# Transposes on TensorE replaced by 32x32 block turns on VectorE, with h sent through DRAM, in a three-stage attention and expert kernel

## The chip, the cores and the metric

One core of one Trainium2 chip. The metric is the device time of one execution in microseconds, the median of several runs. A profiled execution of the same program gives the trace that is read here.

## The reference, cut to what matters

Block-sparse attention (2 batches, 8 heads, 768 positions, heads of 64) gives 1536 tokens of 512 numbers. A gate picks one of eight experts for each token, and the token goes through that expert's two layers. Last comes a dense layer pair with a squared ReLU.

```
logits = x @ w_gate + modality_bias[modality_id]
e_idx  = argmax(logits);  gate_w = softmax(logits)[e_idx]
for e in range(8):
    h = maximum(x[mask] @ w1[e], 0)          # 512 -> 1024
    out[mask] = gate_w[mask] * (h @ w2[e])   # 1024 -> 512
h = maximum(x @ w_in, 0)                     # 512 -> 2048
return h * h @ w_out                         # 2048 -> 512
```

## The kernel before, in words

**Attention** runs over 12 blocks of 128 tokens. Its rows are scattered to DRAM (xs_d), sorted by expert. With these inputs three experts have tokens, in 13 tiles of 128 rows.

**Expert tiles.** Every product is made of three fp32r matmuls: each operand is split into a high part, rounded by a copy on ScalarE (x_hi, h_hi, W), and a low part, the rest, from a subtraction on VectorE (x_lo, h_lo). Layer 1 is 24 matmuls of 512 columns into banks 0 and 1 (lines 1536 to 1538), layer 2 is 24 matmuls into bank 4 (lines 1559 to 1561). Tiles 0 to 2 are written out ahead of the loop, tiles 3 to 12 run in a loop over pairs. TensorE's order in the loop is: layer 1 of tile t; 4 transposes of x for tile t+1 (`x_transpose`, line 1492, from x_in to bank 5); layer 2 of tile t-1; 8 transposes of h for tile t (`h_transpose`, line 1569, banks 2 and 3).

ScalarE's order in a step is: ReLU of the two halves of h (line 673), x_hi of t+1, h_hi twice (line 677), the store of y of tile t-1 (line 688), and last, at some tiles, the splitting of the next weights, whose turn it reads from a table in SBUF (`split_next`; one half of 2 MB at a time, four copies of 1024 columns). VectorE's order: x_lo of t+1, copy of y(t-1) out of bank 4 (line 1179), h_lo twice, low parts of the weights (`low_next`). GpSimd loads the weights, 2 MB at a time, and makes two of a run's eight low parts. SyncE loads x tile by tile (`load_x`). All engines take their instructions in this order and wait on semaphores: `x_t` counts turned x tiles, `ht` turned halves of h, `hh` and `hl` their high and low parts, `relu` the ReLUs, `y` the copies of y, `l1` and `l2` the finished layers.

**Dense layers.** Rows come back from DRAM (ys_d) in three groups of 512. The first group's rows (z) are scaled by the gate weight and turned by 16 TensorE transposes between the last h_transpose and the last expert layer 2 (`part_transposes`). Inside a group, `up(g, f)` is 12 matmuls for 128 of the 2048 hidden columns and `down(g, f)` 12 matmuls back, two steps behind. The next group's z is scaled on VectorE in the middle of a group and turned by 8 transposes after the last `up` and 8 after the next `down` (`z_transpose`, line 1633). 24 more matmuls of `down` end the group, and the four results are copied to o_sb and scattered to the output.

Of the kernel before, what the change touches and what calls it, by code (L numbers as in the profile page):

```python
# [14 lines left out]
P = 128  # L15
# [36 lines left out]
GT = 4  # L52
# [16 lines left out]
AHEAD = 1  # L69
VPITCH = 9 * P  # L70
# [74 lines left out]
def build(nc, a):  # L145
# [26 lines left out]
    cursor["t"] = c_mark + (2 * DM + 2 * DM + FE + 2 * FE + 2 * DM + DM) * 4  # L172
# [96 lines left out]
    x_hi = sb("c", "x_hi", [P, KD, P], F32R)  # L269
    x_lo = sb("c", "x_lo", [P, KD, P], F32R)  # L270
    h_sb = sb("c", "h_sb", [P, FE], F32)
    h_hi = sb("c", "h_hi", [P, KF, P], F32R)
    h_lo = sb("c", "h_lo", [P, KF, P], F32R)
# [8 lines left out]
    z_in = sb("c", "z_in", [P, GT, DM], F32)  # L282
# [9 lines left out]
    z_part = [sb("c", f"z_part{s}", [P, DM], F32) for s in range(2)] + x_in  # L292
    z_hi = sb("c", "z_hi", [P, KD, GT * P], F32R)
    z_lo = sb("c", "z_lo", [P, KD, GT * P], F32R)

# [5 lines left out]
    ys_d = nc.dram_tensor("ys_d", (N + P, DM), F32).ap()  # L301
    meta_d = nc.dram_tensor("meta_d", (N, 2), F32).ap()
# [17 lines left out]
    def Wv(slot, lo, col, n):  # L320
# [10 lines left out]
        raw0 raw1 zfill scat_a x_t x_h x_l l1 relu ht hh hl l2 y sh sla slbv slbp  # L331
        counts both ylast wo_h wo_v zin scale zt zh zl m1 r sqs s_h s_l mo o_a o_v out ofree den_ok""".split()
# [10 lines left out]
    s_part = [nc.alloc_semaphore(f"s_part{j}") for j in range(GT)]  # L343
# [60 lines left out]
    def part_bank(j):  # L404

        return bank[(6, 7, 0, 1)[j]]

    def z_bank(k):

        return bank[6 + k % 2]  # L410

    block = nc.Block()
    with block:

        @block.sync
        def _(sp):
# [69 lines left out]
            def load_x(t, s):  # L486
                row = sp.value_load(table[0:1, bass.ds(t + T_ROW, 1)], min_val=0, max_val=E * EROWS)
                sp.dma_start(x_in[s][:, :], xs_d[bass.ds(row, P), :]).then_inc(s_xs[s], 16)
# [24 lines left out]
            sp.wait_ge(sem["tab"], 1)  # L513
            done = sp.value_load(table[0:1, T_DONE:T_DONE + 1], min_val=LEAST - RECENT, max_val=TILES - RECENT)
            for s in range(2):
                stored = sp.snap(((done + (RECENT - s)) >> 1) * 16)
                sp.wait_ge(s_ys[s], stored)
            sp.wait_ge(sem["metas"], NB * 16)
            for j in range(GT):
                if j == 2:  # L520
                    sp.wait_ge(sem["x_t"], n_t + 1)
                sp.dma_start(z_part[j][:, :], ys_d[j * P:(j + 1) * P, :]).then_inc(s_part[j], 16)
# [7 lines left out]
            sp.sem_inc(sem["ofree"], 1)  # L530
            for g in range(1, GROUPS):
                sp.wait_ge(sem["zt"], g * KD)
                sp.dma_start(z_in[:, :, :], ys_d[g * GT * P:(g + 1) * GT * P, :].rearrange("(j p) d -> p j d", p=P)
                             ).then_inc(sem["zin"], 16)
# [7 lines left out]
        def _(act):  # L542
# [45 lines left out]
            def x_high(t):  # L588
                act.wait_ge(sem["x_t"], t + 1)
                act.activation(x_hi[:, :, :], x_bank(t)[:, :].rearrange("p (k t) -> p k t", k=KD), ACT.Copy  # L590
                               ).then_inc(sem["x_h"], 1)
# [37 lines left out]
            def split_next(t, half):  # L629

                k = act.value_load(table[0:1, bass.ds(t + T_NEXT, 1)], min_val=0, max_val=E)
                with act.If(k > 0):
                    split_w(act.value_load(table[0:1, bass.ds(t + T_NEXT, 1)], min_val=1, max_val=E), half)
# [26 lines left out]
            def parts_high():  # L660
                for j in range(GT):
                    act.wait_ge(sem["zt"], j + 1)
                    act.activation(z_hi[:, :, j * P:(j + 1) * P], part_bank(j)[:, :].rearrange("p (k t) -> p k t", k=KD),
# [1060 lines left out]
```

## Time and the profile before

| what | us |
|---|---|
| median of 3 runs | 521.39 (521.07 to 522.05) |
| profiled execution, its own time | 521.77 |
| span of its instructions | 520.1 |
| TensorE busy | 508.1 (98%) |
| VectorE busy | 225.4 (43%) |
| ScalarE busy | 188.0 (36%) |
| GpSimd busy | 87.1 (17%) |
| mean granted TensorE clock | 0.998 |

Busy shares are averages over the whole span, and the attention, expert and dense stages have different work. The chain that ended last is 95% TensorE.

### The profile page before, as it was taken

To read this page: it belongs to the slowest core of one execution; us is meant where nothing else is said; L and a number is where in the kernel's file an instruction comes from. 1 tells how busy PE (TensorE), PEld (TensorE's weight loads), DVE (VectorE), ACT (ScalarE), POOL (GpSimd) and SP (SyncE) were. 2 spreads that over 40 slices of the span, in tenths; PEclk is the share of its full clock that TensorE was granted. 3 is DMA by queue.
4 is the path that set the end of the run, shared out by engine and by line. 5 is a ranking of instruction groups with operands and counts; after the bars stand their busy time and mean duration, and the time that the engine had idled before them with its cause. 6 is when DMAs were issued, how large, how long until landed. Compare 5 with 4: busy or idle time off the path is not lost.

```text
span 520.1 us, 9415 instructions
## 1 busy us (share of the span) xinstructions
PE 508.1 (98%) x3115; PEld 410.0 (79%) x3117; DVE 225.4 (43%) x440; ACT 188.0 (36%) x355; POOL 87.1 (17%) x110
## 2 busy tenths in 40 slices
PE   8889999999999999999999999999999999999995
PEld 3678788888888888888788888888888888888884
DVE  4787686974323554237632422342242233222221
ACT  1876665243524544225522212331221233122121
POOL 4434335027600223100000000300000020000002
PEclk9999999999999999999999999999999999999999
DMA  8999666384661655521200000400000020000002
GB/s 285 336 290 340 235 220 228 99 285 104 189 216 41 219 204 202 202 82 40 83 1 1 0 1 0 161 0 0 0 0 0 0 81 0 0 0 0 0 0 81
DMA packets 19018, 54.92 MB, mean 106 GB/s; under 512 B 2848, under 2 KB 3120, under 8 KB 18480
## 3 DMA queue, kind: packets, MB, share of 16 engines
q1 hardware_dynamic: 11200, 27.47, 16.6%
q0 software_dynamic: 5200, 23.62, 12.6%
q10 hardware_dynamic: 2592, 3.49, 1.8%
q8 instruction: 15, 0.25, 0.2%
q14 instruction: 11, 0.09, 0.1%
HBM read 42.51 MB, written 12.07 MB: 105 GB/s over the span
## 4 chain that ended last, share of the span: by engine, by line
PE 95%; DVE 3%; issue 1%; ACT 1%; POOL 0%; POOLq 0%; DVEq 0%; ACTq 0%
PE psum L1653 9%; PE psum L1654 9%; PE psum L1652 9%; PE psum L1668 8%; PE psum L1669 8%; PE psum L1670 8%; PE psum L1536 5%; PE psum L1559 5%; PE psum L1538 5%; PE psum L1560 5%; PE psum L1561 5%; PE psum L1537 5%; PE psum L1396 2%; PE psum L1569 2%; PE psum L1371 2%; PE psum L1456 2%
## 5 line engine op out<-in xcount | busy, mean ns | idle before, releaser
L1326 DVE TENSOR_TENSOR sq<-r_sb 128x512 f32<-128x512 f32 x48 | 33.2, 692 | 141.4 <-ACT r_sb L734 137.4
L734 ACT ACTIVATE r_sb<-psum 128x512 f32<-128x512 f32 x48 | 28.7, 597 | 143.7 <-PE psum L1654 143.7
L1668 PE MATMUL psum<-W,s_hi 128*128 128x512 f32 x192 | 75.9, 395 | 0.1
L1653 PE MATMUL psum<-z_lo,W 128*128 128x512 f32 x192 | 75.8, 395 | 0.0
L1654 PE MATMUL psum<-z_hi,W 128*128 128x512 f32 x192 | 75.8, 395 | 0.0
L1652 PE MATMUL psum<-z_hi,W 128*128 128x512 f32 x192 | 75.8, 395 | 0.0
L1669 PE MATMUL psum<-W,s_hi 128*128 128x512 f32 x192 | 75.5, 393 | 0.0
L1670 PE MATMUL psum<-W,s_lo 128*128 128x512 f32 x192 | 75.4, 393 | 0.0
L893 POOL DMA_INDIRECT out<-o_sb,sorted_m x12 | 11.6, 969 | 293.5 <-DVE o_sb L1342 291.6
L1328 DVE TENSOR_TENSOR s_lo<-sq,s_hi 128x512 fp32r<-128x512 f32 x48 | 33.2, 692 | 33.5 <-ACT s_hi L736 33.5
L736 ACT ACTIVATE s_hi<-sq 128x512 fp32r<-128x512 f32 x48 | 30.3, 632 | 41.8 <-DVE sq L1326 41.8
L1668 PEld LDWEIGHTS psum<-W,s_hi 128*128 128x128 f32 x192 | 36.1, 188 | 8.7 <-issue 0.5
L1652 PEld LDWEIGHTS psum<-z_hi,W 128*128 128x128 f32 x192 | 36.0, 188 | 8.7
L1654 PEld LDWEIGHTS psum<-z_hi,W 128*128 128x128 f32 x192 | 36.0, 187 | 8.7
L1653 PEld LDWEIGHTS psum<-z_lo,W 128*128 128x128 f32 x192 | 36.0, 188 | 8.6
L1670 PEld LDWEIGHTS psum<-W,s_lo 128*128 128x128 f32 x192 | 36.1, 188 | 8.2
L1669 PEld LDWEIGHTS psum<-W,s_hi 128*128 128x128 f32 x192 | 36.1, 188 | 8.1
L1536 PE MATMUL psum<-W,x_hi 128*128 (+1 forms) x104 | 42.1, 405 | 0.3 <-DVE x_lo L1018 0.3
L1559 PE MATMUL psum<-W,h_hi 128*128 (+1 forms) x104 | 42.0, 404 | 0.0
L1538 PE MATMUL psum<-W,x_lo 128*128 (+1 forms) x104 | 40.9, 393 | 0.0
L1560 PE MATMUL psum<-W,h_hi 128*128 (+1 forms) x104 | 40.9, 393 | 0.0
L1561 PE MATMUL psum<-W,h_lo 128*128 (+1 forms) x104 | 40.7, 391 | 0.0
(205 smaller groups left out, 729.5 us busy)
## 6 DMA issues: line engine op xcount, KB each, us to landing
raw<-in_w POOLq DMA_DIRECT2D x4, 2048.0 KB, 9.1
raw<-in_w_io POOLq DMA_DIRECT2D x4, 2048.0 KB, 8.2
v_in<-in_v SPq DMA_DIRECT2D x12, 390.0 KB, 12.7
raw<-in_w SPq DMA_DIRECT2D x8, 512.0 KB, 4.3
kT<-in_kT SPq DMA_DIRECT2D x8, 400.0 KB, 7.9
q_in<-in_q SPq DMA_DIRECT2D x12, 256.0 KB, 8.8
X<-in_vT SPq DMA_DIRECT2D x4, 768.0 KB, 11.7
x_in<-xs_d SPq DMA_DIRECT2D x12, 256.0 KB, 2.8
```

Of the source, the lines that this page charges most:

```text
L1326: dve.tensor_tensor(sq[:, :], r_sb[:, :], r_sb[:, :], ALU.mult).then_inc(sem["sqs"], 1)
L1536: pe.matmul(bank[h][:, :], x_hi[:, k, :], wh, start=(k == 0), stop=False)
L1538: ins = pe.matmul(bank[h][:, :], x_lo[:, k, :], wh, start=False, stop=(k == KD - 1))
L1559: pe.matmul(bank[4][:, :], h_of(t)[1][:, k, :], wh, start=(k == 0), stop=False)
L1560: pe.matmul(bank[4][:, :], h_of(t)[1][:, k, :], wl, start=False, stop=False)
L1561: ins = pe.matmul(bank[4][:, :], h_lo[:, k, :], wh, start=False, stop=(k == KF - 1))
L1652: pe.matmul(bank[f % 2][:, :], wh, z_hi[:, k, :], start=(k == 0), stop=False)
L1653: pe.matmul(bank[f % 2][:, :], wh, z_lo[:, k, :], start=False, stop=False)
L1654: ins = pe.matmul(bank[f % 2][:, :], wl, z_hi[:, k, :], start=False, stop=(k == KD - 1))
L1668: pe.matmul(bank[2 + j][:, :], s_hi[f % SBUFS][:, tok], wh, start=(f == 0), stop=False)
L1669: pe.matmul(bank[2 + j][:, :], s_hi[f % SBUFS][:, tok], wl, start=False, stop=False)
L1670: ins = pe.matmul(bank[2 + j][:, :], s_lo[f % SBUFS][:, tok], wh, start=False, stop=(f == KFF - 1))
```

## The change

- **x in the loop** (tiles 4 to 13): the load from xs_d puts quarter q of the columns on partitions 32q to 32q+31, four tokens to a partition (pieces of 512 B). One VectorE instruction turns all 16 blocks of 32x32 into x_w, which lies where x_lo will be. x_hi and x_lo are made from x_w. There is no TensorE transpose.
- **h in the loop** (tiles 3 to 11): after each ReLU half, SyncE writes the half to DRAM (h_d) and reads it back in the other layout (`spread_h`); VectorE turns it into h_w, which lies where h_lo will be; then h_hi and h_lo. The first half may be turned when half of layer 2 of t-1 is through (`l2m`), the second when all of it is. The last tile and tiles 0 to 2 keep TensorE's transposes.
- **Order**: on ScalarE the splitting of weights stands between x_hi and h_hi, and the second-half split waits for layer 2 of t-1. On VectorE the weights' low parts stand before the turn of h, and the copy of y(t-1) after h_lo. Layer 2 alternates between banks 4 and 7 and takes h by halves.
- **z**: loaded in the same layout in four DMAs per group, turned by four VectorE instructions per group after the last `up`, with z_hi and z_lo from the turned copy in SBUF. The gate weight is no longer applied to z; its square (g_sq) scales the last copies to o_sb.
- **Weights**: the rows of w1, w2 and w_in are laid out in another order ahead of the launch, since a turned tile has column 4p+k of its input on partition p. The TensorE transposes that stay read every fourth column accordingly.

```diff
@@ sync
+            def spread_h(t, lap):
+                for h in range(2):
+                    sp.wait_ge(sem["relu"], t * 2 + (h + 1))
+                    sp.dma_start(h_d[h].rearrange("q t f -> t q f"),
+                                 h_sb[:, h * DM:(h + 1) * DM].rearrange("t (q f) -> t q f", q=KD)).then_inc(s_hd[h], 16)
+                for h in range(2):
+                    sp.wait_ge(s_hd[h], lap * 16)
+                    sp.dma_start(h_q[h][:, :], h_d[h].rearrange("q (a j) f -> (q a) (j f)", a=QW)).then_inc(s_hq[h], 16)
...
                     moe_step(t + 1, 0)
+                    spread_h(t, m * 2 + 1)
+                    with sp.If(t + 2 == n_t):
+                        load_parts()
+            def load_z(g, into):
+                for q in range(KD):
+                    sp.dma_start(into[q * QW:(q + 1) * QW, :], quarter(ys_d[g * GT * P:(g + 1) * GT * P, :], q)
+                                 ).then_inc(sem["zin"], 16)
@@ scalar, split_next
+                    k = act.value_load(table[0:1, bass.ds(t + T_NEXT, 1)], min_val=1, max_val=E)
+                    if seconds is not None:
+                        act.wait_ge(sem["l2"], seconds)
+                    split_w(k, half)
@@ scalar, moe_step
                 x_high(t + 1)
+                if not isinstance(t, int):
+                    with act.If(t == last):
+                        parts_high()
+                    split_next(t - 1, 1, t)
+                    split_next(t, 0)
...
+                    with act.If(t < last):
+                        for h in range(2):
+                            act.wait_ge(sem["ht"], t * 2 + (h + 1))
+                            act.activation(h_hi[:, 4 * h:4 * h + 4, :], h_w[:, 4 * h:4 * h + 4, :], ACT.Copy
+                                           ).then_inc(sem["hh"], 1)
...
-                if not isinstance(t, int):
-                    split_next(t - 1, 1)
-                    split_next(t, 0)
@@ vector
+            def x_turn(t, s, lapx):
+                dve.wait_ge(s_xs[s], lapx * 16)
+                dve.wait_ge(sem["l1"], t * 2)
+                dve.transpose(turned(x_w[:, :, :]), blocks(x_in[s][:, :])).then_inc(sem["x_t"], 1)
+
+            def h_turn(t, h, lap):
+                dve.wait_ge(s_hq[h], lap * 16)
+                dve.wait_ge(sem["l2" if h else "l2m"], t)
+                dve.transpose(turned(h_w[:, 4 * h:4 * h + 4, :]), blocks(h_q[h][:, :])).then_inc(sem["ht"], 1)
...
+            def loop_step(t, s, lap):
+                with dve.If(t == last):
+                    parts_turn()
+                x_turn(t + 1, s, lap + 1)
+                x_low(t + 1, True)
+                low_next(t - 1, range(PARTS, PARTS + 2))
+                low_next(t, range(PARTS))
+                with dve.If(t == last):
+                    z_low(0)
+                    h_low(t)
+                with dve.If(t < last):
+                    for h in range(2):
+                        h_turn(t, h, lap * 2 - 1 + s)
+                        h_low(t, (h,), True)
+                dve.wait_ge(s_ys[s], lap * 16 + 16)
+                y_copy(t - 1, y_sb[s], s)
+                with dve.If(t == last):
+                    out_low(range(PARTS))
+                    y_copy(last, y_last, 1 - s)
...
                 with dve.If(g < GROUPS - 1):
-                    z_low(g + 1)
+                    dve.wait_ge(sem["zin"], (g + 2) * (KD * 16))
+                    dve.wait_ge(sem["m1"], g * KFF + KFF)
+                    z_turn(z_in, 0)
+                    for k in range(KD):
+                        if k + 1 < KD:
+                            z_turn(z_in, k + 1)
+                        z_low(g + 1, (k,))
                     dve.wait_ge(sem["mo"], g * GT + (j + 1))
-                    dve.tensor_copy(o_sb[:, j, :], bank[2 + j][:, :]).then_inc(sem["o_v"], 1)
+                    dve.tensor_scalar(o_sb[:, j, :], bank[2 + j][:, :], g_sq[:, bass.ds(g * GT + j, 1)], None, ALU.mult
+                                      ).then_inc(sem["o_v"], 1)
@@ tensor, layer2
+                if not isinstance(t, int) or t > 1 - AHEAD:
+                    pe.wait_ge(sem["y"], t - 1 + AHEAD)
...
+                    if k == KF // 2 - 1:
+                        ins.then_inc(sem["l2m"], 1)
@@ tensor, loop
-            def moe_step(t, s, lapx):
+            def moe_step(t, s):
                 last = []
                 layer1(t, *weights_of(t), between=((KD // 2, lambda: last.extend(weights_of(t - 1))),))
-                x_transpose(t + 1, s, lapx)
-                layer2(t - 1, *last)
-                h_transpose(t)
+                layer2(t - 1, s, *last)
...
-                    if f == KFF - 1:
-                        with pe.If(g < GROUPS - 1):
-                            z_transpose(g + 1, range(2))
```

## Rows read from the trace of the kernel before

**Rows 1.** The page: busy us, share, instructions; busy tenths; granted TensorE clock in tenths.

```profile
PE 508.1 (98%) x3115; PEld 410.0 (79%) x3117; DVE 225.4 (43%) x440; ACT 188.0 (36%) x355; POOL 87.1 (17%) x110
...
PE   8889999999999999999999999999999999999995
...
PEclk9999999999999999999999999999999999999999
```

**Rows 2.** Groups of TensorE: line, op, shapes, count, busy us, mean ns.

```profile
L1569 PE MATMUL psum<-ident,h_sb 128*128 128x128 f32 x104 | 13.5, 272 | 0.0
```

**Rows 3.** Chain that ended last, expert loop: start, us, what.

```profile
116.84 0.44 PE psum L1492 x4
...
154.14 0.44 PE psum L1492 x4
...
160.10 0.87 PE psum L1569 x8
...
172.44 0.87 PE psum L1569 x8
```

**Rows 4.** The same chain at the first border of two groups.

```profile
323.88 0.87 PE psum L1633 x8
327.51 1.03 PE psum L1633 x8
```

**Rows 5.** Timeline at that border.

```profile
325.94 0.69 DVE L1328 TENSOR_TENSOR s_lo<-sq,s_hi 128x512 fp32r<-128x512 f32 x1 [0.70 <-ACT s_hi L736]
```

**Rows 6.** The chain before the last expert layer 2.

```profile
234.13 0.88 PE psum L1569 x8
...
237.14 0.36 PE psum L1559
```

**Rows 7.** Timeline at the same place.

```profile
235.24 1.29 DVE L1013 TENSOR_TENSOR h_lo<-psum,h_hi 128x512 fp32r<-128x512 f32 x2 [0.30 <-ACT h_hi L677]
...
236.36 1.09 ACT L663 ACTIVATE z_hi<-psum 128x512 fp32r<-128x512 f32 x2 [0.66 <-PE psum L1621]
```

**Rows 8.** Timeline of ScalarE, tiles 5 to 7.

```profile
154.67 0.59 ACT L590 ACTIVATE x_hi<-psum 128x512 fp32r<-128x512 f32 x1
160.57 1.09 ACT L677 ACTIVATE h_hi<-psum 128x512 fp32r<-128x512 f32 x2 [5.31 <-PE psum L1569]
161.85 0.35 ACTq L688 DMA_DIRECT2D ys_d<-y_sb  x1
164.54 3.90 ACT L585 ACTIVATE W<-raw 128x1024 f32 x4 [2.88 <-issue]
...
176.37 3.90 ACT L585 ACTIVATE W<-raw 128x1024 f32 x4 [2.37 <-issue]
```

**Rows 9.** Timeline of VectorE, tiles 6 and 7.

```profile
160.20 0.69 DVE L1179 COPY y_sb<-psum 128x512 f32<-128x512 f32 x1 [4.21 <-PE psum L1561]
161.20 1.29 DVE L1013 TENSOR_TENSOR h_lo<-psum,h_hi 128x512 fp32r<-128x512 f32 x2 [0.31 <-ACT h_hi L677]
165.88 4.63 DVE L1005 TENSOR_TENSOR W<-raw,W 128x1024 f32 x4 [3.39 <-ACT W L585]
...
177.77 2.36 DVE L1005 TENSOR_TENSOR W<-raw,W 128x1024 f32 x2 [2.94 <-ACT W L585]
```

**Rows 10.** DMA issues, KB each, us to landing; last line: loads of x_in.

```profile
raw<-in_w POOLq DMA_DIRECT2D x4, 2048.0 KB, 9.1
...
ys_d<-y_last SPq DMA_DIRECT2D x1, 256.0 KB, 2.1
...
DMA to landing us min/median/max: 2.5/2.8/4.1
```

**Rows 11.** Groups of VectorE, columns as in rows 2.

```profile
L1309 DVE TENSOR_SCALAR z_in<-z_in,sorted_m 128x512 f32<-128x512 f32 x8 | 3.3, 481 | 0.0
```

**Rows 12.** Timeline of GpSimd: weight loads in the loop, first and last of six.

```profile
134.99 0.81 POOL L849 DMA_DIRECT2D raw<-in_w  x1 [0.46 <-issue]
...
210.22 0.57 POOL L858 DMA_DIRECT2D raw<-in_w_io  x1 [0.41 <-issue]
```

More of the change, by code:

```diff
@@ L342, in build @@
     s_ys = [nc.alloc_semaphore(f"s_ys{s}") for s in range(2)]
[L343 removed]
+    s_hd = [nc.alloc_semaphore(f"s_hd{h}") for h in range(2)]
+    s_hq = [nc.alloc_semaphore(f"s_hq{h}") for h in range(2)]
     s_wo = [nc.alloc_semaphore(f"s_wor{s}") for s in range(2)]
@@ L487, in load_x, with load_parts @@
                 row = sp.value_load(table[0:1, bass.ds(t + T_ROW, 1)], min_val=0, max_val=E * EROWS)
-                sp.dma_start(x_in[s][:, :], xs_d[bass.ds(row, P), :]).then_inc(s_xs[s], 16)
+                if isinstance(t, int) and t <= SPEC:
+                    sp.dma_start(x_in[s][:, :], xs_d[bass.ds(row, P), :]).then_inc(s_xs[s], 16)
+                else:
+                    sp.dma_start(x_in[s][:, :], xs_d[bass.ds(row, P), :].rearrange("(a j) (q f) -> q a j f", a=QW, f=P)
+                                 ).then_inc(s_xs[s], 16)
+            def spread_h(t, lap):
[10 more added lines that the diff above has]
+                                 ).then_inc(sem["zin"], 16)
+            def load_parts():
+                sp.wait_ge(sem["tab"], 1)
+                done = sp.value_load(table[0:1, T_DONE:T_DONE + 1], min_val=LEAST - RECENT, max_val=TILES - RECENT)
+                for s in range(2):
+                    stored = sp.snap(((done + (RECENT - s)) >> 1) * 16)
+                    sp.wait_ge(s_ys[s], stored)
+                sp.wait_ge(sem["metas"], NB * 16)
+                load_z(0, z_q)
             sp.wait_ge(sem["scat_b"], RGROUPS[2][1] * 16)
@@ L510, in _ @@
                     moe_step(t + 1, 0)
+                    spread_h(t, m * 2 + 1)
+                    with sp.If(t + 2 == n_t):
+                        load_parts()
                     with sp.If(t + 2 < n_t):
                         moe_step(t + 2, 1)
[L513 to L522, printed above, removed]
+                        spread_h(t + 1, m * 2 + 2)
+                        with sp.If(t + 3 == n_t):
+                            load_parts()
             at = sp.value_load(table[0:1, bass.ds(n_t - 1 + T_POS, 1)], min_val=0, max_val=N)
@@ L660, in parts_high @@
             def parts_high():
-                for j in range(GT):
-                    act.wait_ge(sem["zt"], j + 1)
-                    act.activation(z_hi[:, :, j * P:(j + 1) * P], part_bank(j)[:, :].rearrange("p (k t) -> p k t", k=KD),
-                                   ACT.Copy).then_inc(sem["zh"], 1)
+                act.wait_ge(sem["zt"], KD)
+                for k in range(KD):
+                    act.activation(z_hi[:, k, :], z_w[:, k, :], ACT.Copy).then_inc(sem["zh"], 1)
             def moe_step(t, s=None, before=None):
@@ L1552, in layer2 @@
                             do()
-                    if halves and k == KF // 2:
+                    if k == KF // 2:
                         pe.wait_ge(sem["hl"], t * 2 + 2)
```

207 lines of the change are left out of this document (99 added, 108 removed).

## The prediction

> **What bounds the kernel now.** Page first, then the chain, then TensorE's, ScalarE's and VectorE's timelines in the expert loop, then the transfers. The page [rows 1] has TensorE busy for 508.1 us of the span at full granted clock (tenths of 9 throughout: the 2.4 GHz level), VectorE for 225.4, ScalarE for 188.0. The chain stays on TensorE through the loop: between two groups of transposes lie 24 matmuls, 154.58 to 160.10, so a layer is 5.52 us (0.23 per matmul), and a tile is 4 transposes of x (0.44), layer 2 of the tile before, 8 transposes of h (0.87), layer 1: 12.34 us [rows 2, 3]. (Matmul rows of 0.39 overlap; the distance of starts is the price.) Nothing on the other engines is late there: ScalarE and VectorE wait for TensorE (5.31 us before h_hi, 4.21 before the copy of y) [rows 8, 9]. So each TensorE instruction removed is worth its time, as long as what replaces it keeps under TensorE's other work.
>
> **What is removed.** Tiles 3 to 12 run in the loop (13 tiles: 104 transposes of h are 13 times 8 [rows 2]). Ten turns of x go, 10 x 0.44 = 4.4 us; nine of h (tiles 3 to 11; the last tile keeps TensorE's), 9 x 0.87 = 7.8. The 32 transposes of z at the two group borders are 0.87 + 1.03 each border, 2 x 1.90 = 3.8 us [rows 4]; the 16 before the last layer 2 occupy the 2.13 us between the end of h's transposes (235.01) and that layer's start (237.14) [rows 6]. If all that replaces them were hidden: at the last place h_lo's first half ends only at 235.93, so 0.9 of the 2.13 stays as a wait [rows 7], and 4.4 + 7.8 + 1.2 + 3.8 = 17.2 us are saved.
>
> **Group borders.** After the last first-layer matmul of a group TensorE still has 36 matmuls (8.3 us). VectorE must do sq and s_lo (2.8 us after it: 326.63, where the transposes behind those matmuls are through from 323.88 on [rows 4, 5]), then 4 turns and 4 subtractions at some 0.65 us: 8.1 us for all four quarters, while next group's matmuls want them at 8.3, 9.0, 9.7, 10.4. Even turns of 1.2 us fit nearly (10.4). The z rows are asked for a whole group ahead. I count the full 3.8. The factor g squared in the last copies replaces copies of the same shape: nothing.
>
> **The new ring.** The loop is another matter. ScalarE and VectorE work in order, and in ScalarE's order the ReLU of tile t+1 stands behind the store of y(t-1), which waits for VectorE's copy of y(t-1), which now stands behind both halves of h(t): turn, h_hi, h_lo. Those wait for h(t)'s trip through DRAM, which starts at the ReLU of tile t. So from ReLU to ReLU there is a ring that TensorE's 11.0 us per tile (24 + 24 matmuls) doesn't enter. Its prices: x_hi 0.6, and the ReLU, a copy of the same shape, the same [rows 8]; h_hi 0.58 with 0.08 to hand over; h_lo and y copies 0.64 apiece in a row (1.29 for two) [rows 9]. The transfers: 256 KB took 2.1 us out (y_last), 2.5 to 4.1 in, median 2.8 [rows 10]. The write out has pieces of 512 B, which no row shows; bounds 2.1 and 4.1, I take 2.7 for it, near the store with its larger pieces, and 2.7 for the way back. The 32x32 turn isn't shown either: 0.48 (the scale of z_in, SBUF to SBUF) below, 1.2 (the 128x1024 subtraction, 2.36 for two) above [rows 9, 11]; I take 0.64, the in-a-row price of the other 128x512 instructions.
>
> Plain tile, counted from the start of its ReLU: ReLU 0.6, issue 0.15, out 2.7, 0.05, back 2.7, 0.1: h's first half is back at 6.3. Turn 0.64, h_hi 0.66, h_lo 0.72: 8.3. The second half, already there, the same in order: 10.3. Copy of y 11.0; store's issue and the loop's edge (0.1 + 0.35 + 0.5): the next ReLU at **11.9**. TensorE needs 11.0. So each plain tile gets 0.9 later than TensorE's pace, which by itself would take 2.9 us of slack first.
>
> **Tiles that split weights.** Before, the splits stood behind h_hi and the store; now they stand ahead of h_hi on ScalarE and ahead of the turn on VectorE. First half of a run's weights (tiles 6, 8): ReLU pair and x_hi are done at 1.7, the table reads take 2.34 (162.20 to 164.54), and VectorE's fourth part ends 5.97 after the first of ScalarE's starts (164.54 to 170.51) [rows 8, 9]: 10.0. The trip is covered, but then turn, h_hi, h_lo (2.0) twice, copy and edge follow: **15.7**. Second half (tiles 7, 9): reads 1.76, VectorE's two parts end 3.76 after the start: 7.2, ring **12.8**. Tile 3 splits a second half too and ScalarE waits there for layer 2's end at 5.5, then 3.9 of copies: ring 14.9.
>
> Six weight loads of 2 MB (9.1 us each) fall between 134.99 and 218 [rows 10, 12]. An x load issued in such a load took up to 4.1 instead of 2.7. I add 0.6 per transfer, 1.2 per trip, where the trip is what the ring waits for: tiles 4, 5, 11. Bounds 0 and 2.8.
>
> **The sum**, from the end of layer 1 of tile 3. ReLU(3) -0.5; +14.9 tile 3; +13.1 +13.1 tiles 4, 5; +15.7 +12.8 +15.7 +12.8 tiles 6 to 9; +11.9 tile 10: ReLU(11) at 109.5. Tile 11's copy of y ends 11.0 + 1.2 later, 121.7. In the last tile VectorE turns z's four quarters first (2.6), then x of the unused tile 13 (0.74), then ScalarE x_hi (0.7), four z_hi (2.07, as 1.09 for two in [rows 7]), two table reads (1.76), h_hi 0.6, h_lo 0.7: the last layer 2 starts at 130.9. Before, it was 237.14 - 116.84 = 120.3 [rows 3, 6] on the same scale (19 layers of 5.52, 10 x 0.44, 10 x 0.87, 2.13). So +10.6, less 3.8 at the borders: **+6.8 us**. Against the profiled execution's 521.77 (0.4 above the median of 521.39) that is 528.6; I forecast **528.5**.
>
> With every price at its lower bound (2.1 and 2.5 for the trip, no contention, turns 0.48): rings of tiles 4, 5, 10, 11 lose 0.8 each, contention 3.6, 23 turns 0.16 each: 10.5 less, 518. If table reads and the loop's edge run ahead behind ScalarE's work as well (some 0.6 x 5 + 0.3 x 9), 512. Upper: both transfers 4.1 adds 2.8 to four rings, less the 3.6 counted: +8; turns of 1.2 add 23 x 0.56 = 13: 550.
>
> The turns read and write fp32 values 16 bytes apart. Only contiguous 128x512 rows stand in this trace, at 0.48 to 0.69 us [rows 9, 11]. The Trainium skill ("SBUF — State Buffer", Door 1: The DMA port swizzle) says that SBUF serves lines of 16 bytes and that a stream that moves to a new line at each access pays for it; no run here shows it yet. By it the turn lies at the upper bound, and the 48 TensorE transposes that stay, which now read with that step too, would also cost more. That outcome is the second rival.
>
> **The rivals.**
> - *The ring is short* (chance 0.17, other side): trips of 4.6 us and run-ahead reads give 512 to 518; if no ring binds at all, 521.8 - 17.2 = 504.6. For it: the quickest landings are 2.1 and 2.5, and VectorE is idle for over half of a plain tile. Against: splits now stand ahead of h even then, and two rings of over 15 us stay. It decides where the summed rings fall 6.8 us below mine, a plain ring of 11.0 or less with splits of 14.5.
> - *Turns are slow* (0.15): 1.2 us each, 528.6 + 13 = 542; 48 transposes at twice their 0.11 would add 5.
> - *The trip is slow* (0.10): landings near 4 us, 536 to 538.
> - *The gaps let TensorE's clock fall* (0.03): gaps of 1 to 5 us per tile would come; the trace of before has no slice in which TensorE is busy under 0.8 up to the last, so it shows no clock after such gaps [rows 1]. A fall to the 1.2 GHz level would double the following 5.52 us layers: above 550.
> - *Tie by accident* (0.05).
> The forecast itself (528.5, own range 522.5 to 535): 0.50.
>
> **How the numbers follow.** Within 0.2% (1.04 us) is what a measurement of this kernel can't tell from no change. Faster 0.18, same 0.05, slower 0.77. Range 514 to 544: it takes in the short ring at its bounds and the slow turns, and leaves out the fully hidden case and the clock.
>
> **What would show it.** Gaps of TensorE before layer 2 of tiles 4 to 11, ended by h_lo; ReLUs that start 11 to 16 us apart, ended by the store of y or a wait on VectorE; landings of about 2.7 for h_q; a TRANSPOSE row of about 0.65 on VectorE; ScalarE's h_hi idle until a turn. At the borders, up-matmuls with no wait and a group 1.9 us shorter. Wrong if ReLU to ReLU is 11.0 in plain tiles (TensorE still sets the pace), or if the turn is over 1 us.

## The result and the profile after

The changed kernel takes 565.98 us (median of 4 runs, 564.26 to 569.31) against 521.72 for the kernel before on the same chip (521.07 to 523.8): ratio 1.085, 95% interval 1.0817 to 1.0884. Forecast were 528.5, slower, with 514 to 544 as the range. So the direction came as forecast, and the loss is 44 us where 6.8 were counted. Some executions of a kernel take over 1.5% longer than its fastest; the ratios below leave these out, the medians don't.

The page of the changed kernel, cut to what answers to [rows 1]: busy us and share; busy tenths of TensorE; granted clock in tenths; the chain by engine.

```profile
PE 505.8 (90%) x2956; PEld 403.4 (72%) x2957; DVE 267.1 (47%) x469; ACT 190.7 (34%) x355; POOL 88.7 (16%) x110
...
PE   7999999994579775788499999999999999999995
...
PEclk9999999996979797889889999999999999999998
...
PE 61%; DMA 18%; DVE 7%; issue 4%; ACT 4%; ACTq 2%; SPq 1%; DVEq 1%; POOL 0%; POOLq 0%
```

TensorE has 159 instructions fewer than before and is busy only 2.3 us less, because matmuls at a low clock last longer. The damage is in slices 10 to 20 (127 to 282 us), the expert loop: busy tenths of 4 to 8 in all but one of them where [rows 1] has 9, and the granted clock falls in most of them. TensorE's waits in the loop (110 to 290 us; who waited for whom, us in total, times, longest) name one thing:

```profile
PE psum L1640 <- DVE h_lo L1076: 42.1, 8, 9.2
PE psum L1616 <- DVE x_lo L1083: 4.0, 5, 1.1
```

L1640 is the first matmul of layer 2. The chain shows what stands behind h_lo. Tiles 3 and 4 first, then tile 5, in which no weight load runs:

```profile
117.47 0.49 ACT h_sb L718
...
118.52 8.49 DMA h_d<-h_sb
127.03 8.05 DMA h_q<-h_d
135.10 1.14 DVE h_w L1093
136.26 0.64 ACT h_hi L740
...
137.55 0.69 DVE y_sb L1253
138.48 0.34 ACTq L751
...
139.52 0.60 ACT h_sb L718
140.14 8.82 DMA h_d<-h_sb
148.98 6.14 DMA h_q<-h_d
...
162.08 0.61 ACT h_sb L718
162.70 2.35 DMA h_d<-h_sb
165.08 2.60 DMA h_q<-h_d
```

This is the ring of the prediction, link by link: ReLU, out, back, turn, h_hi, h_lo, copy of y, its store, next ReLU. The quiet trip is 2.35 + 2.60 (counted: 2.7 + 2.7). The other two are 16.5 and 15.0. ReLU to ReLU takes 22.1, 22.6, 12.2, 16.2, 15.6, 18.3, 17.6, 16.1 and 12.3 us in tiles 3 to 11: 153.1 together, 123.1 forecast.

The turns of h among VectorE's groups in the loop (columns as in [rows 2]); the ten of x have a mean of 1118 ns:

```profile
L1093 DVE STREAM_TRANSPOSE h_w<-h_q 128x512 f32<-128x512 f32 x18 | 20.1, 1117 | 34.7 <-DMA h_q<-h_d 34.6
```

Stretches of the trace (start and end, us, busy time and count of each engine, granted clock, DMA share, GB/s): the write of tile 3, the layer 2 behind its trip, the writes of tiles 4 and 5, the last layer 2, and the second MLP:

```profile
118.50:127.00 8.50, 7.91 (x35) 6.21 (x34) 4.86 (x5) 4.54 (x5) 6.67 (x7) 1.00 0.51 105
135.40:140.40 5.00, 5.00 (x12) 3.94 (x13) 3.21 (x4) 1.51 (x3) 4.11 (x4) 0.50 0.41 62
140.10:149.00 8.90, 8.39 (x35) 6.52 (x35) 2.53 (x1) 1.02 (x3) 4.39 (x4) 0.96 1.01 366
162.70:165.10 2.40, 2.40 (x12) 1.97 (x11) 0.69 (x1) 0.98 (x2) 0.00 (x0) 1.00 0.57 174
283.00:287.00 4.00, 4.00 (x10) 3.14 (x11) 1.43 (x3) 2.34 (x3) 0.00 (x0) 0.50 0.17 66
300.00:540.00 240.00, 240.00 (x1037) 194.32 (x1036) 80.27 (x111) 63.73 (x104) 7.78 (x8) 1.00 0.05 14
```

Tile 4's long write has the DMA engines full, with two weight loads of 2 MB issued at 137.54 and 144.61. In its first 5.4 us (140.1 to 145.5) the queues moved (packets, MB, share of the engines' time; q0 has GpSimd's loads, q1 SyncE's pieces of h):

```profile
q0 software_dynamic: 399, 1.63, 81.3%
...
q1 hardware_dynamic: 60, 0.03, 1.9%
```

From 145.5 to 149 q1 moves 0.49 MB. So the write hardly moves before 1.6 MB of the loads have moved. Tile 8's is the same (0.01 MB in the first 5.0 us), and tile 10's too (none in the first 3.4). Tile 3's is another case: q1 moves 0.48 MB in 4.0 us and needs another 4.5 for 0.12 MB, at 29 GB/s in all, while GpSimd's scatters are on their way.

And the last tile, where z is turned ahead of h (the chain of the changed kernel; it answers to [rows 6]):

```profile
265.75 5.91 DMA z_q<-ys_d
271.68 0.06 DVE z_w L1320
...
272.73 3.05 DVE z_w L1320 x3
...
281.81 0.61 DVE h_lo L1076
...
282.86 0.79 PE psum L1640
```

The last layer 2 starts at 282.86, 45.7 us later than in [rows 6]. From there to the end of the span the changed kernel needs 281.2, the one before 283.0. So all of the loss lies ahead of this point.

### The profile page after: what moved, and what is told of

The parts are those of the page before. It is cut to its first block, busy times and chain, and to the rows that moved or that the text cites. A ratio compares the mean times of both kernels' runs of the same rounds, so it can differ in the third digit from the quotient of the medians.

```text
span 564.1 us, 9300 instructions
## 1 busy us (share of the span) xinstructions
PE 505.8 (90%) x2956; PEld 403.4 (72%) x2957; DVE 267.1 (47%) x469; ACT 190.7 (34%) x355; POOL 88.7 (16%) x110
## 4 chain that ended last, share of the span: by engine, by line
PE 61%; DMA 18%; DVE 7%; issue 4%; ACT 4%; ACTq 2%; SPq 1%; DVEq 1%; POOL 0%; POOLq 0%
PE psum L1717 8%; PE psum L1718 8%; PE psum L1716 8%; PE psum L1733 8%; PE psum L1732 8%; PE psum L1734 8%; DMA h_d<-h_sb 7%; DMA h_q<-h_d 4%; DVE h_w L1093 3%; DMA q_in<-in_q 3%; PE psum L1640 2%; ACT h_hi L740 2%; PE psum L1641 1%; PE psum L1642 1%; PE psum L1450 1%
## 5 line engine op out<-in xcount | busy, mean ns | idle before, releaser
L1640 PE MATMUL psum<-W,h_hi 128*128 (+1 forms) x104 | 48.4, 465 | 42.1 <-DVE h_lo L1076 42.1
L794 ACT ACTIVATE r_sb<-psum 128x512 f32<-128x512 f32 x48 | 28.7, 597 | 145.8 <-PE psum L1718 139.6
L954 POOL DMA_INDIRECT out<-o_sb,sorted_m x12 | 11.6, 966 | 309.5 <-DVE o_sb L1420 307.0
L1640 PEld LDWEIGHTS psum<-W,h_hi 128*128 128x128 f32 x104 | 23.0, 221 | 51.1 <-issue 45.9
L1641 PE MATMUL psum<-W,h_hi 128*128 (+1 forms) x104 | 46.0, 442 | 0.0
L1642 PE MATMUL psum<-W,h_lo 128*128 (+1 forms) x104 | 45.6, 438 | 0.0
## 6 DMA issues: line engine op xcount, KB each, us to landing
v_in<-in_v SPq DMA_DIRECT2D x12, 390.0 KB, 12.2
```

Source lines behind the costliest of these rows:

```text
L1640: pe.matmul(y, h_of(t)[1][:, k, :], wh, start=(k == 0), stop=False)
L1641: pe.matmul(y, h_of(t)[1][:, k, :], wl, start=False, stop=False)
L1642: ins = pe.matmul(y, h_lo[:, k, :], wh, start=False, stop=(k == KF - 1))
```

## The experiments

Each kernel is the changed one with the edit shown, unless said otherwise. The ratio is to the kernel before, run in turn with it on the same chip. Where effects are compared in us, the ratio is taken times 521.7; the changed kernel is then 566.0.

**The trip and the traffic beside it**

*Loads cut.*

```diff
-                    pool.dma_start(raw[:, part]...(k f)..., w[bass.ds(e, 1)]...)
+                    pool.dma_start(raw[:, part]...(k f)...[:, 0:1, :], w[bass.ds(e, 1), :, 0:1, :]...)
```

> Leaves out seven eighths (layer-2 halves) or three quarters (layer-1 halves) of each weight load inside the loop, so later experts and the dense pair compute with stale weights; nothing else differs from the changed kernel. Theory A (the loop's time is the sum of rings from ReLU to ReLU, and a ring is long where h's trip through DRAM runs beside another transfer): the trips of tiles 4, 8, 9, 10 fall from 8 to 15 us to about 5 us, and the time from 566 to about 548. The trip of tile 3 stays near 16 us, since the weight load beside it ended at 122.2 and the metadata scatters run to 135. Rival B (the weight loads don't matter, TensorE's fallen clock or VectorE's turns cost the time): 562 to 566.

549.06 us, ratio 1.0519 (1.0468 to 1.0571): 17 us less than the changed kernel. Tile 3's trip in its chain:

```profile
122.05 5.54 DMA h_d<-h_sb
127.61 5.05 DMA h_q<-h_d
```

10.6 instead of 16.5, where it was expected to stay near 16, and still twice the quiet one, though only a quarter or an eighth of a half's weights moves.

*No scatters.* The metadata scatters of GpSimd, which in the changed kernel run from 112.7 to 129.7, are replaced by one plain copy.

> Leaves out the 12 scatters of gate weight and token number to DRAM and their read back; the unsorted values are copied instead, so rows leave with another token's place and weight. Theory A (any transfer beside it lengthens the trip): the trip of tile 3, 16.5 us beside these scatters of 8-byte pieces, falls by some 8 us, and the time to about 558. Rival E (tile 3's trip is long because the weight load of 109.1 is still on its way): 564 to 566.

559.17 us, 1.0719 (1.068 to 1.0757), 7 us less. Tile 3's trip is 4.71 + 7.60: 4.2 less, where some 8 were expected. The run isn't clean. The loads that GpSimd issues behind the scatters, at 137.54 and 144.61 in the changed kernel, are issued at 123.96 and 135.16 here, so one of them falls on tile 3's way back, and the largest gain is in tile 4, where no scatters ran (from ReLU to ReLU 16.8 for 22.6). Both the loads and the scatters lengthen the trip of tile 3, by 6 and 4 us in one trace each; how the 7 us divide between the scatters themselves and the earlier loads isn't shown.

*x loads in four parts.*

```diff
-                    sp.dma_start(x_in[s][:, :], xs_d[bass.ds(row, P), :].rearrange("(a j) (q f) -> q a j f", a=QW, f=P)
-                                 ).then_inc(s_xs[s], 16)
+                    for q in range(KD):
+                        sp.dma_start(x_in[s][q * QW:(q + 1) * QW, :], quarter(xs_d[bass.ds(row, P), :], q)
+                                     ).then_inc(s_xs[s], 16)
```

> The x loads of the loop, in the changed kernel one transfer with 4 as its outermost dimension, are issued as four, one per quarter; the bytes are the same. In the changed kernel the DMA share stands at 0.25 for 8.3 us behind such a load (4 engines of 16) and at 0.55 to 0.72 in h's own transfers. Theory F (these 8 us on four engines lie before h's write in part of the tiles and hold it up beside a weight load): the long trips of tiles 4, 9 and 10 shrink by 2 to 4 us each, 555 to 560. Rival (weight loads alone make the trips long): 564 to 567.

567.47 us, 1.0845 (1.0814 to 1.0876): no change, so nothing shows that the x loads delay the trip. The time from ReLU to ReLU is spread otherwise, though: 28.7 us in tile 3 (22.1 in the changed kernel) and 19.3 in tile 4 (22.6). VectorE's and GpSimd's timelines in tile 3 show a second thing that the prediction hadn't; behind them stand two rows of the kernel before:

```profile
139.50 5.29 DVE L1077 TENSOR_TENSOR h_lo<-h_w,h_hi 128x512 fp32r<-128x512 f32 x1 [0.70 <-ACT h_hi L741]
139.53 4.70 POOL L891 TENSOR_TENSOR W<-raw,W 128x1024 f32 x2
```

```profile
179.67 5.09 POOL L829 TENSOR_TENSOR W<-raw,W 128x1024 f32 x2 [7.56 <-ACT W L585]
181.76 0.69 DVE L1018 TENSOR_TENSOR x_lo<-psum,x_hi 128x512 fp32r<-128x512 f32 x1 [1.63 <-ACT x_hi L590]
```

A subtraction of VectorE with both inputs in SBUF that starts beside one of GpSimd's ends some 0.55 us after it or its successor has ended (here 144.79, GpSimd's pair 144.23), and takes 0.8 to 5.3 us instead of 0.69. One with an input in PSUM takes 0.69 there, too. The change moved h and x from PSUM to SBUF. In the trace of the changed kernel three of the 18 h_lo and one of the ten x_lo are lengthened so, by 4.4 us together and up to 1.8 each, in the steps of tiles 4, 7 and 9; in the kernel before none is.

*Larger pieces out.*

```diff
-                    sp.dma_start(h_d[h].rearrange("q t f -> t q f"), h_sb[...].rearrange("t (q f) -> t q f", q=KD))
+                    sp.dma_start(h_d[h], h_sb[:, h * DM:(h + 1) * DM])
...
-                    sp.dma_start(h_q[h][:, :], h_d[h].rearrange("q (a j) f -> (q a) (j f)", a=QW))
+                    sp.dma_start(h_q[h][:, :], h_d[h].rearrange("(a j) (q f) -> q a j f", a=QW, f=P))
```

> h is written to DRAM in pieces of 2 KB (one row of a half) and read back in pieces of 512 B, the other way round than in the changed kernel; the result is the same. Theory A1 (a transfer in small pieces gets few turns beside another queue's large pieces, whichever way it goes): the long landings move from the write to the read, time 560 to 568. Rival A2 (it is writing 512 B pieces to DRAM that is slow): the trips beside weight loads shrink by some 4 us each, 548 to 555.

598.84 us, 1.1471 (1.1424 to 1.1517): 32 us worse, against both theories. Its chain in a tile without a weight load, and the stretch of the read-back by itself (columns as in the stretches above):

```profile
178.16 2.21 DMA h_d<-h_sb
180.39 8.37 DMA h_q<-h_d
```

```profile
180.40:189.00 8.60, 5.85 (x26) 4.51 (x25) 2.04 (x3) 0.63 (x1) 0.00 (x0) 1.00 0.25 71
```

With nothing beside it the write in whole rows is about as fast as the one in 512 B pieces (2.35), so there the size of the pieces isn't the price. The read now has an outermost dimension of 4 and uses a quarter of the DMA engines (share 0.25, 71 GB/s) for 8.4 us. The Trainium skill (DMA: Bandwidth & Descriptors, Rules for kernel authors) says that an outermost dimension smaller than 16 confines a transfer to at most that many engines; the 0.25 agrees. The run says little of contention, since it brought in a cost of its own; its writes in whole rows still took 4.3 to 9.9 us in tiles 4 and 7 to 10.

*No trip.* h is turned from where ReLU leaves it; its values then stand in other places.

```diff
-                dve.wait_ge(s_hq[h], lap * 16)
+                dve.wait_ge(sem["relu"], t * 2 + (h + 1))
                 dve.wait_ge(sem["l2" if h else "l2m"], t)
-                dve.transpose(turned(h_w[:, 4 * h:4 * h + 4, :]), blocks(h_q[h][:, :])).then_inc(sem["ht"], 1)
+                dve.transpose(turned(h_w[:, 4 * h:4 * h + 4, :]), blocks(h_sb[:, h * DM:(h + 1) * DM])).then_inc(sem["ht"], 1)
```

> Leaves out h's way through DRAM: VectorE turns h's blocks straight from h_sb (the blocks are then in the wrong partitions, so h is wrong), all waits and the order of the engines stay. Theory A: plain rings fall under TensorE's 11.0 us, only the rings with a first-half weight split (16 us) and the last tile still cost; about 521 us. Rival C (VectorE with turns of 1.12 us is the bound whatever the transfers do): 540 or more.

532.3 us, 1.0203 (1.0173 to 1.0233). The trip is worth 34 of the 44 us. But 521 was expected, and 10.6 us of loss remain without it. TensorE's waits in its loop:

```profile
PE psum L1634 <- DVE h_lo L1070: 14.4, 5, 5.0
```

Its rings are 10.6 to 10.8 in three tiles and 12.1 in tile 4, but 14.5 to 15.7 in the five tiles that split weights. That ring doesn't contain the trip.

*Splits behind h.* The same, with `split_next` and `low_next` put behind h_hi and h_lo.

```diff
                 x_low(t + 1, True)
-                low_next(t - 1, range(PARTS, PARTS + 2))
-                low_next(t, range(PARTS))
...
                         h_low(t, (h,), True)
+                low_next(t - 1, range(PARTS, PARTS + 2))
+                low_next(t, range(PARTS))
                 dve.wait_ge(s_ys[s], lap * 16 + 16)
```

> The changed kernel without the trip through DRAM (h turned from where ReLU writes it, so its values stand in other places), and with the splits of the next weights put behind the turns and splits of h on ScalarE and VectorE rather than ahead of them. It tells what the 10.5 us are that the kernel without the trip still lost. Theory (the order of the queues: a first-half split stands ahead of h_hi and h_lo and makes the ring 15.7 rather than 10.6 to 12): four such tiles by some 3.4, so 13 to 14 less than without the trip alone, 518 to 521, with the last ReLU of the loop near 227. Rival (TensorE needs the split halves as early as the turned h, so the wait moves from h_lo to the split weights): within 3 of the kernel without the trip, 529 to 533, with waits of layer 1 on the weights' low parts in the rows.

529.55 us, 1.012 (1.0074 to 1.0165): by the ratio 4 us less, where the theory said 13 and the rival under 3 (529 to 533). TensorE's waits:

```profile
PE psum L1610 <- DVE x_lo L1077: 8.7, 2, 4.7
PE psum L1634 <- DVE h_lo L1070: 3.4, 1, 3.4
```

The wait for h_lo is gone from the loop (the 3.4 left are at the last tile). Of the 9.3 us that it had there, 6.6 came back one step later, in front of layer 1, for x_lo (8.7 for 2.1). VectorE's timeline in such a tile says why:

```profile
185.53 1.12 DVE L1082 STREAM_TRANSPOSE x_w<-x_in 128x512 f32<-128x512 f32 x1
188.29 1.92 DVE L1077 TENSOR_TENSOR x_lo<-x_w,x_hi 128x512 fp32r<-128x512 f32 x1 [1.64 <-ACT x_hi L628]
190.13 1.09 DVE L1087 STREAM_TRANSPOSE h_w<-h_sb 128x512 f32<-128x512 f32 x1
...
197.20 4.64 DVE L1060 TENSOR_TENSOR W<-raw,W 128x1024 f32 x4 [2.17 <-ACT W L619]
201.75 0.68 DVE L1247 COPY y_sb<-psum 128x512 f32<-128x512 f32 x1
202.35 1.11 DVE L1082 STREAM_TRANSPOSE x_w<-x_in 128x512 f32<-128x512 f32 x1
```

A tile with a first-half split has x's turn and split, h's two turns and splits, four low parts and a copy of y on VectorE, with hand-overs to ScalarE between. From turn of x to turn of x that row of work takes 16.8 us (1.2 of them because x_lo runs beside GpSimd), and TensorE needs 11. In either order the tiles with a first-half split take 15.7 to 17.2. The rival had its number, but the waits are for x_lo and not for the weights' low parts, so neither theory had this: the order chiefly chooses where it is felt.

**VectorE's part of the ring**

*Copy of y ahead.*

```diff
+                dve.wait_ge(s_ys[s], lap * 16 + 16)
+                y_copy(t - 1, y_sb[s], s)
                 with dve.If(t < last):
                     for h in range(2):
                         h_turn(t, h, lap * 2 - 1 + s)
                         h_low(t, (h,), True)
-                dve.wait_ge(s_ys[s], lap * 16 + 16)
-                y_copy(t - 1, y_sb[s], s)
```

> The copy of y of tile t-1 stands ahead of the turn of h instead of behind h_lo; the result is the same. Theory A: ScalarE's store no longer waits for the second h_lo and the copy, 1.4 to 1.8 us less per ring, nine rings: about 552. Rival D (the ring closes only through the transfers and the buffer of h, not through ScalarE's store): 566 unchanged.

561.07 us, 1.075 (1.0722 to 1.0778): 5 us, where 14 were expected. It takes the tail off the ring in plain tiles (11.0 and 10.7 for 12.2 and 12.3), but the waits for h_lo stay at 41.4 us, and tiles 3 and 4 still take over 21 us. The nine rings are 7.5 shorter in its trace, and the last tile, up to layer 2, 1.4 longer (13.8). The h_hi of a tile stands ahead of the next ReLU on ScalarE in any case, and that waits for the trip. In two places its chain goes over TensorE instead: h_lo, layer 2, and then what waits for that layer (once the turn of the next tile's h, once a second-half split). So cutting the ring at the copy of y leaves others of nearly the same length.

*Contiguous turns.* x and h are turned block by block in place, so their values stand in other places; z's turns stay.

```diff
-                dve.transpose(turned(h_w[:, 4 * h:4 * h + 4, :]), blocks(h_q[h][:, :])).then_inc(sem["ht"], 1)
+                dve.transpose(h_w[:, 4 * h:4 * h + 4, :].rearrange("p k (n c) -> p (k n) c", c=QW),
+                              h_q[h][:, :].rearrange("p (n c) -> p n c", c=QW)).then_inc(sem["ht"], 1)
```

> The turns of x and h on VectorE read and write contiguous values instead of one value every 16 bytes (the elements then land in other places, so the result is wrong); instruction count, sizes and waits are the changed kernel's, z's turns stay as they are. If the 16-byte step costs: a turn falls from 1.12 to some 0.65 us, two turns per ring and one more in the last tile, about 9 us less: 556. If the block turn itself costs 1.12 us for 512 columns: 566.

561.24 us, 1.0782 (1.0712 to 1.0851): 3.5 us less, with an interval of 0 to 7, where 9 were expected. The turn by itself is clear:

```profile
L1094 DVE STREAM_TRANSPOSE h_w<-h_q 128x512 f32<-128x512 f32 x18 | 12.7, 707 | 36.5 <-DMA h_q<-h_d 36.5
...
L1322 DVE STREAM_TRANSPOSE z_w<-z_q 128x512 f32<-128x512 f32 x4 | 4.1, 1101 | 2.9 <-DMA z_q<-ys_d 2.9
```

Contiguous 0.71, with the 16-byte step 1.12: the step costs 0.41. The 0.64 of the prediction was near the contiguous one. The rule that the prediction cited from the Trainium skill (SBUF — State Buffer, Door 1) agrees in direction.

**The clock**

*Fillers.* Twenty bf16 matmuls of 512 columns that nobody uses, before each layer 2 of the loop.

```diff
+                for _ in range(20):
+                    pe.matmul(bank[6]..., fill[:, 0:P], wide(fill[:, :], 1, 2), start=True, stop=True)
                 layer2(t - 1, s, *last)
```

> 20 bf16 matmuls of 512 columns (0.23 us each, 4.6 us) on a spare bank stand between layer 1 and layer 2 of every tile of the loop; the result is the same. They keep TensorE at work for half of the long gaps. Theory A (TensorE isn't in the ring, so a slow layer 2 mostly costs slack): granted clock above 0.98 in the loop, but the time moves by less than 5 us, 561 to 570. Rival B (the 16 us by which the layer 2 matmuls are longer add to the time): 550 to 553.

569.87 us, 1.0904 (1.0833 to 1.0975), by the ratio 3 more than the changed kernel; the mean granted clock is 0.99 instead of 0.955. The first of the three matmuls of its layer 2, with TensorE's wait:

```profile
L1642 PE MATMUL psum<-W,h_hi 128*128 (+1 forms) x85 | 37.4, 440 | 12.3 <-DVE h_lo L1078 12.3
```

TensorE waits 30 us less (the fillers stand in the gaps), its matmuls are half to two thirds of the way back to the price of the kernel before (475, 452 and 447 ns became 440, 412 and 413; before 403, 394 and 391), and the time doesn't fall. The rival's 550 to 553 is out: most of what layer 2 loses to the clock is slack. It isn't quite nothing. The second-half split waits for layer 2, and in tile 7 of the changed kernel the chain runs through that layer (186.42 to 194.77), with its first matmuls 0.43 apart; the split's low parts end 1.1 us later than forecast. There the fillers take as much time as they can give back, so this run doesn't measure it.

**The versions with h on TensorE**

*Hybrid.* h goes back to TensorE's transposes and the order of the kernel before; x and z stay on VectorE.

> h goes back to TensorE's transposes and the weight splits back behind the store, x and z stay turned on VectorE. Theory A: no ring is left, 4.4 us of x transposes and 3.8 us of z transposes are saved and some of the 2.1 us before the last layer 2: 512 to 514. Rival C (a turn of 1.12 us per tile on VectorE delays the splits or x_lo): 519 to 523.

522.79 us, 0.999 (0.9958 to 1.0023): even, the number of the rival. Its chain at the last tile (z's load lands at 227.4):

```profile
229.35 2.05 DVE z_w L1306 x2
231.41 0.98 DVE x_w L1078
...
237.82 0.49 PE psum L1626
```

The last layer 2 starts at 237.82, later than the 237.14 of [rows 6]: z's turns stand before x and h on VectorE. The loop ahead of it gained nothing either: the last ReLU is at 227.68 against 227.53. A plain tile takes 11.96 instead of 12.34, so a turn of x does save some 0.4, but the first tiles of the loop give it back, where TensorE waits 0.9 for x_lo and 1.6 for nothing that the profile shows.

*Order of the last tile.* The hybrid, with z turned and split after h.

```diff
                 with dve.If(t == last):
-                    parts_turn()
...
                 h_low(t)
                 with dve.If(t == last):
+                    parts_turn()
+                    z_low(0)
                     out_low(range(PARTS))
```

> As h1_hybrid, but in the last tile h_hi and h_lo stand ahead of the turn and the split of z's first group. In h1_hybrid the last layer 2 started at 237.8 (before: 237.1), after a wait of 3.0 us on h_lo behind z's turns, whose rows landed only at 227.4, and TensorE's clock fell after it. Theory G (x and z on VectorE save what was counted, 4.4 and 3.8 us, and h1_hybrid gave it back at this one place): 515 to 518. Rival C (the turns of x cost elsewhere): 521 to 523.

527.05 us, 1.0081 (1.0034 to 1.0129): slower than the hybrid, where 515 to 518 were expected. Layer 2 does start sooner, 8.4 us after the last ReLU instead of 10.1. Then TensorE waits 0.8 for z_lo and 4.2 for the first ReLU of the dense layers, which ScalarE starts late:

```profile
254.93 0.60 ACT L781 ACTIVATE r_sb<-psum 128x512 f32<-128x512 f32 x1 [5.82 <-DVE g_sq L1372]
```

g_sq is the gate's square, one instruction of 0.17 us. ScalarE waits for it ahead of all dense layers, and VectorE makes it only behind z, the weights' low parts and the last copy of y. After this gap the granted clock is 0.50 (255.6 to 260.0). The same wait of 5.8 stands in the next two versions. So the theory isn't refuted: these runs measure the place of g_sq along with the order, and one with g_sq made earlier wasn't run.

*The same with x on TensorE.*

> As h3_order, but x too is turned by TensorE as in the kernel before; only z's turns are on VectorE. Theory G: 4.4 us more than h3_order, 519 to 522. Rival (x's turns on VectorE give nothing, since splits and x_lo wait behind them): equal to h3_order within 1 us.

528.45 us, 1.0119 (1.0067 to 1.0172). Against 527.05 of the run before, x on VectorE is worth 1.4 us, within the spread of both.

*The same with x loads in four parts.*

> h3_order with the x loads by quarters. With no trip in the ring, x loads are covered by a whole tile: equal to h3_order within 1 us (both theories); over 2 us less would say that the 8 us loads also hold up the store of y and z's rows at the end.

525.56 us, 1.0049 (1.0013 to 1.0086): the interval overlaps that of the version without it. Not settled.

*Borders alone.* The kernel before, with nothing of the loop touched:

```diff
-                with dve.If(g < GROUPS - 1):
-                    z_low(g + 1)
+                with dve.If(g < GROUPS - 1):
+                    dve.wait_ge(sem["zin"], (g + 1) * (KD * 16))
+                    dve.wait_ge(sem["m1"], g * KFF + KFF)
+                    z_turn(z_in, 0)
+                    ...
...
-                with pe.If(g < GROUPS - 1):
-                    z_transpose(g + 1, range(2, KD))
```

> The kernel before with one part of the change only: z at the two borders of the second MLP is turned on VectorE, with the gate put on the output as its square; the first group's z, x and h stay on TensorE as before. Theory (a border lost 1.9 us of TensorE time before and loses none now, wherever the loop stands): before minus 3.8, so 517.6 where before is 521.4, and the border waits of the second MLP gone from the rows; the time of the loop the same within 0.5. Rival (what the changed kernel gained behind the loop came from its slower start, its later clock or its output loads standing further ahead, not from the turns): no change, 521.4. A second rival (the turns, 1.1 us each rather than 0.64, are late at the border and TensorE waits for the third and fourth): before minus 1 or less, 520.4 or above.

518.38 us against 522.55, 0.9931 (0.9909 to 0.9953): 3.6 us faster than the kernel before; the theory said 3.8. The page of this version, and TensorE's only wait behind the loop:

```profile
PE 504.1 (98%) x3084; PEld 407.2 (79%) x3085; DVE 228.5 (44%) x437; ACT 188.7 (37%) x355; POOL 87.1 (17%) x110
```

```profile
PE psum L1650 <- ACT r_sb L744: 0.7, 1, 0.7
```

Thirty-one instructions fewer on TensorE than in [rows 1] (32 transposes went), 4 us less busy, and no wait for z at a border. It beats both kernels.

*Borders and x.* The same, with x of the loop's tiles on VectorE as well.

> The run of the borders alone, and x of the loop's tiles also turned on VectorE, in the place where its split stood. Theory (x is worth the 1.4 us by which two earlier hybrids differed, since VectorE's turn of 1.1 us stands in the way of the y copy and so of the next layer 2): 1 to 2 us faster than the borders alone, so about 516.2. Rival (the term as predicted, 0.44 to 0.47 of TensorE for each of nine tiles, 4.2): 513.4. A second rival (the x load in its four-level form, or the turn in the last tile, is late): slower than the borders alone, 518 or above.

518.72 us, 0.9915 (0.9884 to 0.9946). By the ratio 0.8 us better than the borders alone, by the median 0.3 worse; the intervals overlap. So x on VectorE is worth nothing that these runs can tell, and not the 4.2 of the rival. A plain tile takes 11.88 against 12.33, the 0.44 of the prediction; but tile 2's ReLU, ahead of the loop, is 1.0 later (108.54 for 107.59), tile 3's ring 0.7 longer, and TensorE waits 1.1 for x_lo and 0.9 for nothing shown, where it waited for nothing. Two x_lo, now read from SBUF, take 1.07 beside GpSimd's subtractions. From tile 3's ReLU to the last one it is 108.5 against 109.1, and the last ReLU is at 227.85 against 227.32.

## Why the prediction was wrong

The ring and the direction were right; the term for contention on the trip was taken at 1.2 us, where tiles 3 and 4 show 10 and more. Point by point.

- **What bounds the kernel before**: right. TensorE set the pace, and the borders alone gave back 3.6 of the 3.8 us counted.
- **The new ring**: right. The chain runs through its links in the predicted order, and where nothing disturbs the trip it takes 12.2 and 12.3 us (11.9 and the 1.2 added for contention: 13.1 forecast). That this nears 11.9 is in part luck: two turns are 1.0 dearer than taken, and the quiet trip is 0.45 shorter.
- **Contention on the trip is the step that failed.** "I add 0.6 per transfer", with 2.8 as the upper bound per trip, from x loads that took up to 4.1 instead of 2.8. h's transfers took 8.49 and 8.05, 8.82 and 6.14: 10.0 to 11.6 us above the quiet trip. Tile 3 came out 7.3 above the forecast, tile 4 9.5, tile 10 4.3. Without most of the loads the kernel is 17 us faster, without the scatters (and with earlier loads) 7, without the trip 34. The prediction read the contention from loads that nobody waits for, of the larger pieces, and counted it only where "the trip is what the ring waits for": tiles 3 and 6 to 9 were taken as covered by the splits. The trip outgrew that cover. The scatters, which fall on tile 3, weren't counted at all.
- **The turn**: 0.64 taken, 1.12 measured, inside the bounds of 0.48 to 1.2; the prediction had named a turn over 1 us as a sign of being wrong. By the prediction's own working that is 23 x 0.48 = 11 us, an upper value, since part of the turns of h lies under a late trip. The runs with contiguous turns gave 3.5 us for 0.41 per turn.
- **Splits ahead of h**: 15.7 forecast for a first-half tile, 16.2 and 18.3 measured with the trip, 15.7 in both without. Right in size. A second-half tile was put at 12.8 and took 15.6 in tile 7 and 17.6 in tile 9, 14.5 and 14.6 without the trip. In tile 7 the low parts end 1.1 late, because the split waits for layer 2; the turns add 1.0, and two h_lo beside GpSimd 0.7. The prediction had that wait in tile 3 alone and had nothing for GpSimd. In the run without the trip the first-half tiles' price was expected, but 521 left out what the second-half tiles cost. Putting the splits behind h moves two thirds of the wait to x_lo.
- **The last tile**: from its ReLU to the last layer 2, 8.3 us by the prediction's terms, 12.4 measured. The four turns take 4.1 and not 2.6, and z's load, 5.9 us long, ends 1.2 us after the ReLU started (271.68 against 270.47), so they start only there.
- **The sum** closes: the rings are 30.0 longer than forecast, the last tile 4.1, tile 3's ReLU is 1.0 later than put; together 35.1, and 10.6 were forecast: 45.7, as the rows have it.
- **The clock** was a rival with a chance of 0.03, priced above 550. It fell to the lower level after gaps of the loop (0.50 in 135.4 to 140.4), which the rival named as its cause, but it isn't what most of the time comes from: at a mean of 0.99 the kernel was no faster. It costs up to 1.1 us in tile 7, and it costs where TensorE is the bound, at the last layer 2: some eleven matmuls stand 0.43 apart instead of 0.23 (0.50 in 283 to 287), 2.2 us. With the 3.8 counted at the borders that leaves 1.6 of the 1.8 by which the changed kernel is faster behind the loop.
- **The rivals**: "turns are slow" and "the trip is slow" came true together, and the second far beyond the "near 4 us" for which it was priced. The range took each by itself.

Left open: what holds up tile 3's trip, where the DMA engines were only half busy (0.51, 105 GB/s), and which of the moved and missing transfers gave the 7 us of the run without scatters. In tiles 4, 8 and 10 the queues' rows show the write of h waiting behind a load.

## What to carry to other kernels

Before a value goes through DRAM inside a loop, look at what else moves in the same microseconds, and price the trip by a transfer that runs beside a large load and whose landing somebody waits for. If there is none in the trace, the upper bound is not a few tenths but several times the quiet value (over 3 times here, 16.5 for 4.95). Take a trade apart by place: here the same substitution gained 3.6 us at the borders, where VectorE is idle and the data is early, nothing in sum for x, and lost over 40 in the loop. Count an engine's work per tile in its heaviest tile, not on average: VectorE is busy for 47% of the span, and yet its row of work in a first-half tile, with the hand-overs to ScalarE, takes 16.8 us where TensorE needs 11. And when an operand moves from PSUM to SBUF, look at what GpSimd does in the same microseconds.

## What the runs showed of the hardware

- A 256 KB write in 512 B pieces takes 2.35 us quiet, nearly as one in 2 KB pieces does (2.21); issued during a 2 MB load from GpSimd it took 5.8 to 8.8 (tiles 4, 8 and 10), and in the first 3.4 to 5.4 us of that at most 0.03 MB of it moved.
- A VectorE subtraction of 128x512 with both inputs in SBUF takes 0.69 us alone. Started beside GpSimd's subtraction of 128x1024 it ends some 0.55 us after that or the next one: 0.8 to 5.3 us. With an input in PSUM it takes 0.69 beside it, too.
- A 256 KB read whose outermost dimension is 4 takes 8.4 us at a DMA share of 0.25, the usual form 2.6.
- VectorE's fp32 turn of 128x512 by 32x32 blocks takes 0.71 us contiguous and 1.12 with a step of 16 bytes.
- After gaps of several us (7.4 ahead of the layer 2 at 135.35) TensorE's granted clock is 0.50, the 1.2 GHz level, and matmuls come 0.43 apart instead of 0.23. It shows in the mean of matmul rows (475 ns for 403) without being the cause of most of the time.
